# Routing work moved to other steps, and the first batch's keys loaded in longer rows and put in order by products with the identity

## The reference

```python
# q, k, v: (2, 8, 768, 64), block 32, window 16, nb = 24
k_sum = k.reshape(B, H, nb, block, D).max(axis=3)
v_sum = v.reshape(B, H, nb, block, D).mean(axis=3)
scores_l = scale * q @ k^T, kept only where |i - j| < window
scores_s = scale * q @ k_sum^T + log(block)
a = softmax([scores_l, scores_s]);  x = a @ [v, v_sum]      # -> (1536, 512)
logits = x @ w_gate                                         # 8 experts, argmax picks one
out[mask] = gate * (relu(x[mask] @ w1[e]) @ w2[e])          # for each expert e
h = x @ w_in;  g = max(0.01 * h, h);  result = g @ w_out    # on all 1536 rows
```

## Time and profile before

| | |
|---|---|
| Time, median of 3 runs | 532.45 us (530.99 to 537.22) |
| The profiled execution | 535.45 us, its span 533.7 us |
| PE busy | 512.9 us, 96% of the span |
| DVE, ACT, POOL busy | 264.5, 240.4, 102.9 us |
| Mean granted clock of TensorE | 0.975 of full |
| Attention's steps | 19.4 to 107.0 us of the span |

### The profile page before, as it was taken

How to read it: one execution, slowest core, us unless ns; L and a number is a source line. 1 busy time by engine, 2 the same in 40 slices (tenths; PEclk the granted TensorE clock), 3 DMA queues, 4 the chain that set the end, 5 groups by cost and what they waited for, 6 DMA issues and landing times.

```text
span 533.7 us, 9199 instructions
## 1 busy us (share of the span) xinstructions
PE 512.9 (96%) x3231; PEld 425.7 (80%) x3232; DVE 264.5 (50%) x530; ACT 240.4 (45%) x509; POOL 102.9 (19%) x174
## 2 busy tenths in 40 slices
PE   5799998899999999999999999999999999999996
PEld 5578786798888888888788888888888888888885
DVE  2758785558264441145066247536426734723731
ACT  4668675552253451235156246325425613623610
POOL 6125403425223101100230000140000024000011
PEclk9889997699999999999999999999999999999999
DMA  9999969101837453234142430550640325040001
GB/s 194 224 214 226 221 145 377 56 21 32 302 105 215 117 182 119 88 111 177 54 183 81 164 149 6 193 197 0 225 155 13 120 81 192 0 157 0 0 20 59
DMA packets 74145, 69.04 MB, mean 129 GB/s; under 512 B 47232, under 2 KB 49280, under 8 KB 74112
## 3 DMA queue, kind: packets, MB, share of 16 engines
q1 hardware_dynamic: 64128, 54.16, 35.1%
q0 software_dynamic: 3584, 10.50, 6.3%
q10 hardware_dynamic: 6400, 3.94, 2.7%
HBM read 58.62 MB, written 9.97 MB: 129 GB/s over the span
## 4 chain that ended last, share of the span: by engine, by line
PE 76%; DVE 1%; issue 0%; POOLq 0%; ACT 0%
PE psum L1864 12%; PE psum L1862 12%; PE psum L1863 12%; PE psum L1787 11%; PE psum L1789 11%; PE psum L1788 11%; PE psum L1726 2%; PE psum L1849 1%; PE psum L1840 1%; PE psum L1841 1%; PE psum L1842 1%; PE psum L1850 1%; PE psum L1851 1%; PE psum L1829 0%; DVE hot_row L1310 0%
## 5 line engine op out<-in xcount | busy, mean ns | idle before, releaser
L1787 PE MATMUL psum<-xT_hi,w_hi 128*128 128x512 f32 (+1 forms) x288 | 111.4, 387 | 0.6 <-issue 0.6
L1788 PE MATMUL psum<-xT_lo,w_hi 128*128 128x512 f32 (+1 forms) x288 | 110.5, 384 | 0.0
L1789 PE MATMUL psum<-xT_hi,w_lo 128*128 128x512 f32 (+1 forms) x288 | 110.4, 383 | 0.0
L1862 PE MATMUL psum<-w_hi,h_hi 128*128 128x512 f32 x280 | 109.9, 393 | 0.0
L1864 PE MATMUL psum<-w_hi,h_lo 128*128 128x512 f32 x280 | 109.0, 389 | 0.0
L1863 PE MATMUL psum<-w_lo,h_hi 128*128 128x512 f32 x280 | 109.0, 389 | 0.0
L1434 DVE TENSOR_TENSOR h_full<-psum,h_small 128x512 f32<-128x512 f32 x48 | 33.2, 692 | 75.1 <-ACT h_small L959 73.4
L959 ACT ACTIVATE h_small<-psum 128x512 f32<-128x512 f32 x48 | 28.7, 598 | 88.8 <-PE psum L1789 58.2
L1787 PEld LDWEIGHTS psum<-xT_hi,w_hi 128*128 128x128 f32 x288 | 54.3, 188 | 11.0 <-issue 1.0
L1789 PEld LDWEIGHTS psum<-xT_hi,w_lo 128*128 128x128 f32 x288 | 54.2, 188 | 10.1
L1788 PEld LDWEIGHTS psum<-xT_lo,w_hi 128*128 128x128 f32 x288 | 54.2, 188 | 9.9
(11 more groups left out here) (241 smaller groups left out, 610.1 us busy)
## 6 DMA issues: line engine op xcount, KB each, us to landing
w_raw<-in_moe_w_in SPq DMA_DIRECT2D x12, 1024.0 KB
w_raw<-in_moe_w_out SPq DMA_DIRECT2D x6, 2048.0 KB
w_raw<-in_moe_w SPq DMA_DIRECT2D x6, 1024.0 KB
w_raw<-in_moe_w SPq DMA_DIRECT2D x3, 2048.0 KB
x_rows_sb<-y_rows SPq DMA_DIRECT2D x12, 256.5 KB, 7.9
q_nat<-in_q SPq DMA_DIRECT2D x12, 256.0 KB, 5.9
x_rows<-x_cur ACTq DMA_DIRECT2D x12, 256.0 KB, 4.4
vw_first<-in_v SPq DMA_DIRECT2D x10, 192.0 KB, 5.5
```

Of the source, the lines that this page charges most:

```text
L1787: mm(h, w1_hi[:, c, cols], xT_hi[:, c, 0:n], start=(c == 0), stop=False)
L1788: mm(h, w1_hi[:, c, cols], xT_lo[:, c, 0:n], start=False, stop=False)
L1789: last = mm(h, w1_lo[:, c, cols], xT_hi[:, c, 0:n], start=False, stop=(c == KD - 1))
L1862: mm(y_ps[s % 2], h_hi[:, c, rows], w2_hi[:, c, :], start=(c == 0), stop=False)
```

## The change

Three edits. **Keys of the first batch.** A transfer now holds half of the rows of four heads with three neighbouring rows in a partition, so that 768 B lie together in place of 256 B; there are four transfers, not six. A piece is put in order by six products with the identity (two heads, three rows), where it was three transposes: each product takes 64 columns of `k_first` as its stationary side and writes 64 partitions, with every third column as its target. Each pair of pieces waits for its own transfer alone. **Keys of the second batch.** Their first half is started ahead of the strips of tile 1 and of `w_gate`. **Routing.** `first_hots` is cut in two: its four small operations (`first_rests`) stay in step 17, `hot_row` goes to step 18, behind that step's `normalise` and `softmax`. The inversion goes from step 18 to 19, the copy of its result to `normalise(19)`, and `keep_tokens` right behind that, ahead of the step's `softmax`. `keep_homes` and `new_order` go to step 22, where DVE has no `softmax` left.

```diff
-        k_first = att("k_first", [P, 2, KJ, H, D])
+        k_first = att("k_first", [P, 2, H, KJ * D])
...
+            def load_first_k(half, g):
+                heads = slice(g * HG, (g + 1) * HG)
+                sp.dma_start(k_first[:, half, heads, :],
+                             k[0, heads, half * KHALF:(half + 1) * KHALF, :].rearrange("h (p j) d -> p h (j d)", j=KJ),
+                             ).then_inc(k_first_loaded[half][g], 16)
...
-            load_k(0, 0, [0, 2])
-            load_k(0, 1, [0])
+            load_first_k(0, 0)
+            load_first_k(1, 0)
...
             load_q(2)
+            load_k(0)
             load_strips(1)
             sp.dma_start(w_gate[:], moe_w_gate.rearrange("(c p) e -> p c e", p=P)).then_inc(gate_loaded, 16)
-            load_k(1, 0)
...
-            load_k(0, 1)
+            load_first_k(0, 1)
             act.wait_ge(ident_ready, 1)
             nc.scalar.copy(spare_sb[:], ident[:, 0:1])
-            load_k(1, 1)
-            load_k(1, 2)
+            load_first_k(1, 1)
...
-                if n == ROUTE_STEP + 4:
+                if n == ROUTE_STEP + 5:
                     dve.wait_ge(inverted, 1)
...
-            def first_hots():
+            def first_rests():
...
+            def first_hots():
+                dve.wait_ge(route_step, step[0])
                 tt(hot_row[:, 0:QT, :], iota_p[:].unsqueeze(1).to_broadcast([P, QT, P]),
...
+                if n == ROUTE_STEP + 6:
+                    dve.wait_ge(route_step, step[0])
+                    keep_tokens(0, SUB0)
...
                 if n == ROUTE_STEP + 3:
+                    first_rests()
+                if n == ROUTE_STEP + 4:
                     first_hots()
-                if n == ROUTE_STEP + 5:
-                    dve.wait_ge(route_step, step[0])
-                    keep_tokens(0, SUB0)
-                if n == ROUTE_STEP + 6:
+                if n == UNITS - 2:
                     keep_homes(0, SUB0, first_seat[:])
-                if n == ROUTE_STEP + 7:
                     new_order()
...
+                    pe.wait_ge(k_first_loaded[half][pr // 2], 16)
+                    by_row = kt_ps[m].rearrange("p (r j) -> p j r", j=KJ)
+                    for j in range(KJ):
+                        for sub in range(2):
+                            last = mm(by_row[sub * D:(sub + 1) * D, j, :],
+                                      k_first[:, half, 2 * pr + sub, j * D:(j + 1) * D], ident[:], start=True, stop=True)
...
-                if n == ROUTE_STEP + 4:
+                if n == ROUTE_STEP + 5:
                     pe.wait_ge(hot_row_ready, 1)
```

More of the change, by code:

```diff
@@ L236, in build @@
         assert max(att_end[0], moe_end[0]) <= LAST_BYTE
-        k_nat = [k_first, k_second]
         kw = [kw_first, kw_second]
@@ L278, in build @@
         routing_consts = sem("routing_consts")
-        k_loaded = [[sem(f"k_loaded{b}{half}") for half in range(2)] for b in range(B)]
+        k_first_loaded = [[sem(f"k_first_loaded{half}{g}") for g in range(2)] for half in range(2)]
+        k_loaded = [sem(f"k_loaded{half}") for half in range(2)]
         vn_loaded = [sem(f"vn_loaded{half}") for half in range(2)]
@@ L397, in load_strips, with load_k @@
                                  v[b, :, lo:hi, :].rearrange("h p d -> p h d")).then_inc(v_loaded[t], 16)
-            def load_k(b, half, tiles=range(KJ)):
-                for j in tiles:
+            def load_first_k(half, g):
[3 more added lines that the diff above has]
+                             ).then_inc(k_first_loaded[half][g], 16)
+            def load_k(half):
+                for j in range(KJ):
                     rows = slice((half * KJ + j) * P, (half * KJ + j + 1) * P)
-                    sp.dma_start(k_nat[b][:, half, j], k[b, :, rows, :].rearrange("h p d -> p h d")).then_inc(k_loaded[b][half], 16)
+                    sp.dma_start(k_second[:, half, j], k[1, :, rows, :].rearrange("h p d -> p h d")).then_inc(k_loaded[half], 16)
             def load_v():
@@ L833, in _, with load_first_k @@
         def _(act):
-            def load_k(half, j):
-                rows = slice((half * KJ + j) * P, (half * KJ + j + 1) * P)
-                act.dma_start(k_nat[0][:, half, j], k[0, :, rows, :].rearrange("h p d -> p h d")).then_inc(k_loaded[0][half], 16)
+            def load_first_k(half, g):
+                heads = slice(g * HG, (g + 1) * HG)
+                act.dma_start(k_first[:, half, heads, :],
+                              k[0, heads, half * KHALF:(half + 1) * KHALF, :].rearrange("h (p j) d -> p h (j d)", j=KJ),
+                              ).then_inc(k_first_loaded[half][g], 16)
             def copy_kt(m):
@@ L1280, in first_hots @@
                 chain(stt(out=first_row[:, 0], in0=past[:, :, 1], scalar=-float(P), in1=rank[:, 0:QT, 0], op0=ALU.mult, op1=ALU.add))
-                chain(stt(out=first_row[:, 1], in0=past[:, :, 2], scalar=-float(P), in1=first_row[:, 0], op0=ALU.mult, op1=ALU.add))
+                stt(out=first_row[:, 1], in0=past[:, :, 2], scalar=-float(P), in1=first_row[:, 0],
+                    op0=ALU.mult, op1=ALU.add).then_inc(route_step, 1)
+                step[0] += 1
+            def first_hots():
+                dve.wait_ge(route_step, step[0])
                 tt(hot_row[:, 0:QT, :], iota_p[:].unsqueeze(1).to_broadcast([P, QT, P]),
@@ L1584, in transpose_k @@
                 b, half, pr = piece(m)
[L1585 removed]
                 if b:
+                    pe.wait_ge(k_loaded[half], 16 * KJ)
                     pe.wait_ge(q_ready, 2 + (m - PIECES + K_STEP) // 2)
@@ L1591, in transpose_k @@
                     pe.wait_ge(ksum_maxed, before)
-                for j in range(KJ):
-                    last = nc.tensor.transpose(kt_ps[m][:, j * P:(j + 1) * P],
-                                               k_nat[b][:, half, j, 2 * pr:2 * pr + 2, :], ident[:])
+                if b:
+                    for j in range(KJ):
+                        last = nc.tensor.transpose(kt_ps[m][:, j * P:(j + 1) * P],
+                                                   k_second[:, half, j, 2 * pr:2 * pr + 2, :], ident[:])
+                else:
+                    pe.wait_ge(k_first_loaded[half][pr // 2], 16)
+                    by_row = kt_ps[m].rearrange("p (r j) -> p j r", j=KJ)
+                    for j in range(KJ):
+                        for sub in range(2):
+                            last = mm(by_row[sub * D:(sub + 1) * D, j, :],
+                                      k_first[:, half, 2 * pr + sub, j * D:(j + 1) * D], ident[:], start=True, stop=True)
                 last.then_inc(kt_transposed, 1)
```

3 lines of the change are left out of this document (1 added, 2 removed).

## The result

| | before | after |
|---|---|---|
| Time, median of 20 runs each | 533.29 us (530.99 to 537.22) | 529.92 us (525.61 to 534.75) |
| Profiled execution, span | 535.45, 533.7 us | 532.81, 531.1 us |
| PE busy | 512.9 us | 513.3 us |
| Mean granted clock, profiled | 0.975 | 0.984 |

The ratio is 0.9923, 95% interval 0.9898 to 0.9948: 0.8% faster, some 4.1 us, where 1.5% was forecast (524.5 of 532.45). The ratio leaves out one slow run of the change (534.75 us); the two medians alone are 3.4 us apart. The change works, at half its forecast size or a little less.

The account below looks back on a forecast made before the run. PE, busy 96% behind 108 us, was taken to lose time ahead of that through waits and half clock, with the start bound by transfers. 535.45 - 2.6 (start) - 7.3 (routing) = 525.5 us, taken as 524.5 for the median; range 521 to 530.5.

Parts of the forecast that it names:

- 7.3 us.: Routing, steps 17 to 22: shorter waits and full clock start the experts at 99.7 in place of 107.03 us.
- The start gives 4.3 - 1.7 = 2.6 us: Start to query tile 4: PE gains 4.3 us there, less 1.7 for one expected slow stretch.
- The queue, 2.4 us.: First keys' transfers: 4.7 in place of 7.1 us, so everything behind them on the queue comes 2.4 us earlier.
- The products.: First keys on PE: 56 ns a product record, 0.67 us a piece, keys ending at 11.4 us (12.0 before).
- k_second: Second keys: landing at 23.0 in place of 27.8 us, a wait of 0.8 staying, 4.8 us gained there.
- three cases of five: Start: how often a wait as long as query tile 4's was followed by a slow stretch; one of 3.4 us counted.
- its wait 0.4 in place of 1.73: Routing, last waited transpose_x: it comes at 92.9 in place of 98.42 us, waiting 0.4 us.
- Of 8.6 us 1.8 go: From the last waited transpose_x to the experts: full clock saves 1.8 us, not half, as ACT and DVE work stays.
- (1): Rival: the clock still falls behind shorter waits, so routing gives only the waits, 2.4 us: 530.4 us; chance 0.18.
- (2): Rival: the start gives nothing, longer rows no faster or query tile 4 as late as before: 528.2 us; chance 0.13.
- (3): Rival: first keys' products run unpaired at the lower clock, 213 ns a record, making it slower: 535.7 us; chance 0.05.
- (4): Rival: no slow stretch at query tile 4: 523.8 us; chance 0.14.

Follow-up runs that it names:

- e1: Kernel before with the routing edit alone; 531.07 us, ratio 0.9950 to before.
- e9: Kernel before plus 72 tiny products that compute nothing, in PE's waits ahead of 15 us; 528.28 us, ratio 0.9954 to before.
- e6: Changed kernel without its routing edit (first keys and second keys only); 529.98 us, ratio 0.9945 to before.
- e17: The changed kernel measured again, as a control on the same chip; 528.80 us, ratio 0.9883 to before.
- e13: The changed kernel measured again, beside other variants on one chip; 526.44 us, ratio 0.9918 to before.
- e10: Changed kernel with v_rows loaded in halves and the transfers behind the second held until x_ready is 9; 523.16 us, ratio 0.9852 to before.
- e14: The kernel of e10 again, beside the changed kernel on one chip; 523.30 us, ratio 0.9862 to before.
- e2: Kernel before with the first-keys edit alone (longer rows, products with the identity); 531.22 us, ratio 0.9958 to before.
- e4: Changed kernel with v_rows in two transfers, the first ahead of the strips of tile 4, nothing held; 529.73 us, ratio 0.9931 to before.
- e8: Changed kernel with eight products of the identity ahead of PE's wait for x_cur in step 22; 528.24 us, ratio 0.9907 to before.

## Why the prediction was right or wrong

**Right in direction, twice too large in size.** Two terms of the sum failed.

**"7.3 us." for routing.** Alone it gave 2.6 us (e1, 0.50%). The term was priced on the half-clock stretches of before's one profile, and behind step 18 that profile has more of them than any other. In every profile the time from the experts' start to the end is 426 to 427 us, so what differs lies ahead of them. "Wanted" is the start of `transpose_x` of step 18 less its wait; times in us:

| profiled run | wanted | from there to the experts | of that at half clock |
|---|---|---|---|
| before | 80.87 | 26.2 | 16.2 |
| e9, no routing edit | 81.32 | 20.2 | 3.4 |
| e6, no routing edit | 78.30 | 23.3 | 10.2 |
| e1, routing alone | 82.37 | 22.5 | 10.1 |
| the change | 83.81 | 20.8 | 6.4 |
| the change, e17 | 83.46 | 21.7 | 6.8 |
| the change, e13 | 79.72 | 19.2 | 3.4 |
| e10, strips held | 76.99 | 19.1 | 2.5 |
| e14, strips held | 78.86 | 18.7 | 0 |

The forecast was that the third column falls by 7.3, from 26.2 to 18.9. e9 has 6.0 of these without the edit. Take off half of the last column, as an estimate of what half clock costs, and the three without the edit need 18.1 to 18.5 us, the six with it 17.4 to 18.7: the shorter waits themselves are worth 1 us or less. What the edit does beyond that it does by the clock, and there the mechanism was right: behind a wait of 1.62 us in step 18 the clock fell within 2 us in four profiles of five (not in e2), behind 0.62 us in none of fifteen. At step 22 it was wrong in the executions with late reports, where the wait stays at 1.75 to 2.4 us. For the median run the mean clock gives the size: 0.982 for before beside e1 to e4 is some 19 us at half clock, 0.988 for the change some 13, so 6 us less, worth 3 us at most. The forecast took away stretches worth more than twice that.

**"The start gives 4.3 - 1.7 = 2.6 us".** PE did arrive 4.2 us earlier at query tile 4, but in the profiled pair the start ended 2.9 us behind, for a reason that no rival named: I costed the added products by their time and the moved transfers by each other's, and never by PE's own instructions, which come over the same DMA engines. That e6, the start's two edits alone, gave 0.55%, 2.9 us, and so agrees with 2.6, is luck: it holds a gap (1.41 us in its profile) that no term has.

With the packet out of the way (e10, e14) the ratio is 0.985 to 0.986, the forecast's. That too is partly luck: there the start gives more than its term ("wanted" at 77.0 and 78.9 us for 80.9 to 82.4 where the start is as before) and makes up for routing.

- **The queue, 2.4 us.** Right: query tiles 0 and 1 landed at 9.47 and 10.61 (11.79, 12.88). `v_nat` at 15.75 was right for 15 parts of 16; the last came at 17.74, so the first `weighted_v` gained 0.8 us, not 3.0.
- **The products.** 57 ns for a forecast 56, keys done at 11.6 for 11.4. By the rule of the Trainium skill's "TensorE: Matmul & The Clock Gate", section "Terms", they would have ended at 16.3 us, an estimate from its factor of four. The trace doesn't agree: 8 pieces in 5.46 us are 0.68 a piece, against 0.49 for three transposes in step 3 and on, far from four times.
- **`k_second`.** Landed at 24.90 for 23.0, its wait 0.54 for 0.8, the gain there 2.85 for 4.8. The slow stretches at 15.7 and 29.4 us were gone in this run, and so 4.2 us were reached at query tile 4 by another way than I wrote: no wait of 2.2 us, no slow stretch. In e2, e8, e10 and others a stretch of 3.4 us came back near 18 us.
- **Routing, the parts.** The wait in step 18 is 0.62 for 0.75 and the clock stays up to 98 us: right. The term "its wait 0.4 in place of 1.73" is mis-sized in the profiled run (1.85) and right in e13 (0.35). "Of 8.6 us 1.8 go": at full clock 3.1 go (5.5 us in e6, e8 and e9), and in the change at half clock 0.9. What is late next, I said, is the gather: e13 waits 0.84 us for it.
- **The median.** "If the median run has fewer slow stretches, they are ones that the change removes": not so. Over the 20 runs of the change the time goes with the mean clock, from 525.61 us at 0.997 to 534.75 at 0.975. Half-clock stretches come in other places each run, in before as well.
- **A wait that I read over.** "Ahead of the last three stand waits": ahead of the first slow stretch stood one too, 1.97 us for `q_cur` at 14.56 us in before's timeline, so "three cases of five" was four of six.
- **Rivals.** (1), the clock still falls behind shorter waits, came nearest in time (530.4; its 2.4 us for routing against e1's 2.6) and not in mechanism: it didn't fall behind the wait of 0.62 us. (2) and (3) didn't happen. (4) did, for query tile 4.

The fastest kernel of the study is the change with the strips held, 523.2 us where before has 530.5 to 531.9.

## What to carry to other kernels

Before adding small instructions to an engine, or arriving earlier behind a large transfer, count the engine's instructions and look in the trace for the instruction packets: here they came late while the DMA engines were full of data, and a gap ended by "issue" that stood at the same instruction count in several variants was one that came too late. Holding back a transfer that isn't needed yet can be worth more than starting it early. When edits that are good alone don't add up, look for what all of them bring nearer; and price half-clock stretches by what several runs show, not by one profile. A control that changes no more than the engine's records (e9) told more of the forecast than the change's own profile.

## What the runs showed of the hardware that was not expected

An instruction packet of 16,384 bytes took 0.9 to 2.0 us. Where PE ran out, it went on 2.3 to 3.0 us behind the packet's start, and one part of a transfer that the packet fell into landed up to 2.6 us behind the other 15. PE's completions were reported 0.9 to 2.6 us late while POOL issued indirect gathers, in some executions and not in others, on one and the same chip. And a kernel with 72 products that compute nothing, in waits at the start, was 0.46% faster (0.13 to 0.80), with a mean clock of 0.995 in place of 0.986.
